# Half of a down-projection as three float32r products, with the low part finished by an adding transfer, and a last unit of work done by halves

## The reference, cut to what matters

```
attn = causal 7-tap filter over the sequence, softmaxed taps per head       # 8192 tokens x 192
h = attn @ moe_w_in                # 192 -> 2048
g = h * (1 / (1 + exp(-1.702 * h)))
x2 = g @ moe_w_out                 # 2048 -> 192
h = x2 @ moe2_w_in                 # 192 -> 2048
P = a0 + a1*h + a2*h^2 + a3*h^3
Q = 1 + |b0|*|h| + |b1|*h^2
out = (P / (Q + 1e-6)) @ moe2_w_out   # 2048 -> 192, float32
```

## Time and profile before

| | |
|---|---|
| device time, median of 3 | 1360.77 us (1360.70 to 1365.94) |
| the profiled execution's own time | 1360.97 us |
| its span in the trace | 1358.7 us |
| PE / DVE / ACT / POOL busy | 97 / 82 / 71 / 24 % |
| granted TensorE clock, mean | 0.995 |

### The profile page before, as it was taken

The page is one execution under the profiler, slowest core; times in us unless marked ns, Lnnn a source line. Parts: engine busy times, 40 slices in busy tenths (PEclk is TensorE's granted clock), DMA queues, the critical chain, the costliest instruction groups (busy, mean ns, idle before and its releaser), DMA issues. The chain is left out here.

```text
span 1358.7 us, 14959 instructions
## 1 busy us (share of the span) xinstructions
PE 1315.6 (97%) x4806; PEld 696.6 (51%) x4806; DVE 1115.3 (82%) x1225; ACT 967.3 (71%) x1145; POOL 323.0 (24%) x148
## 2 busy tenths in 40 slices
PE   5999999999999999999999999999999999999885
PEld 3445555555555555555555555555555555555441
DVE  4468888888888888888988888898888888877895
ACT  4357777777767777777777777777777777777684
POOL 2312222222222222222222222222222222222222
PEclk9999999999999999999999999999999999999899
DMA  7200000000000000000000000000000000000000
GB/s 191 73 0 12 1 12 13 1 24 1 12 13 0 23 0 24 0 12 12 0 24 0 23 0 12 13 0 23 0 24 1 12 1 0 13 1 12 0 12 12
DMA packets 32904, 20.55 MB, mean 15 GB/s; under 512 B 10321, under 2 KB 30801, under 8 KB 32849
## 3 DMA queue, kind: packets, MB, share of 16 engines
q1 hardware_dynamic: 32372, 19.93, 5.2%
q10 hardware_dynamic: 477, 0.01, 0.0%
HBM read 13.64 MB, written 6.29 MB: 15 GB/s over the span
## 5 line engine op out<-in xcount | busy, mean ns | idle before, releaser
L751 POOL TENSOR_TENSOR work<-work 128x1024 f32<-128x1024 f32 x128 | 303.3, 2370 | 987.4 <-ACT work L483 935.9
L284 PE MATMUL acc_a<-g,down 128*128 128x512 f32 x1024 | 476.6, 606 | 0.0
L284 PEld LDWEIGHTS acc_a<-g,down 128*128 128x128 f32 x1024 | 183.1, 189 | 291.7 <-issue 291.7
L290 PE MATMUL acc_b<-g,down 128*64 128x512 f32 x992 | 255.1, 606 | 17.6 <-DVE g L652 15.9
L641 DVE TENSOR_TENSOR work<-work,h 128x1024 f32<-128x1024 f32 x128 | 156.4, 1222 | 136.4 <-ACT work L483 135.6
L470 ACT ACTIVATE work<-h,par 128x1024 f32<-128x1024 f32 x128 | 142.7, 1115 | 173.9 <-PE h L278 172.8
L510 ACT ACTIVATE work<-work 128x1024 f32<-128x1024 f32 x128 | 135.9, 1062 | 157.2 <-POOL work L751 156.8
L270 PE MATMUL h<-x_a_hi,up_a_hi 128*128 128x512 f32 x512 | 234.5, 458 | 7.6 <-DVE x_a_lo L655 4.7
L271 PE MATMUL h<-x_a_lo,up_a_hi 128*128 128x512 f32 x512 | 201.3, 393 | 0.0
L272 PE MATMUL h<-x_a_hi,up_a_lo 128*128 128x512 f32 x512 | 200.9, 392 | 0.0
L273 PE MATMUL h<-x_b,up_b_hi 128*128 128x512 f32 x512 | 200.2, 391 | 0.0
(11 more groups left out here) (89 smaller groups left out, 961.0 us busy)
## 6 DMA issues: line engine op xcount, KB each, us to landing
out<-y_out SPq DMA_DIRECT2D x16, 384.0 KB, 2.5
x_in_a<-in_x SPq DMA_DIRECT2D x16, 256.0 KB, 2.8
down<-in_moe_w_out SPq DMA_DIRECT2D x8, 384.0 KB, 6.2
x_in_b<-in_x SPq DMA_DIRECT2D x32, 64.0 KB, 2.4
work<-in_moe_w_in SPq DMA_DIRECT2D x8, 256.0 KB, 4.4
work<-in_moe_w_in SPq DMA_DIRECT2D x16, 128.0 KB, 4.8
wts<-in_weight ACTq DMA_DIRECT2D x2, 0.4 KB
wts<-in_weight SPq DMA_DIRECT2D x2, 1.3 KB
```

Of the source, the lines that this page charges most:

```text
L284: last = mm(l.acc_a[:], l.down[:, f, 0:P], l.g[:, slot, k, :], start=f == 0, stop=f == STEPS - 1)
L290: return mm(acc_b[l.acc_row:l.acc_row + DB, :], l.down[:, f, P:D], l.g[:, slot, k, :], start=f == 0, stop=f == STEPS - 1)
L751: tt(m, sq[(s - LAG_RATIO) % 2], seed, ALU.mult).then_inc(m_ready, 1)
```

## The change

Three things change.

Layer 1's down-product into `acc_a` keeps its first unit (of the two in a duo) in float32, and makes of the second unit three float32r products. The weights' high part, its negative and the negative low part are made once. For the activations ACT makes, right after the function `g`, two copies of minus the rounded second unit, into `g_lo` and `g_nhi`. POOL then begins a transfer that adds the unrounded `g` onto `g_lo`, which leaves the low part there. A one-element multiply into `spare` stands ahead of the transfer on POOL. PE waits for that transfer before the first of these products. Tile 0's duos stay as they were.

The last duo of layer 2 is done in halves of 512 columns, with DVE in POOL's place for `m`, and `down_b` starts with the first half. Three idle matmuls stand on PE ahead of it.

The last tile's read-out is spread: `acc_b` is read as soon as it is done, DVE reads `acc_a`, the second half of the transposes has a bank of its own, DVE copies that half, and the store is two stores.

```diff
@@ pe
+            def down_a_split(d, slot):
+                acc = L1.acc_a[:]
+                mm(acc, L1.down[:, 2 * d, 0:P], L1.g[:, slot, 0, :], start=d == 0, stop=False)
+                mm(acc, down_nhi[:, d, :], g_nhi[:, slot, :], start=False, stop=False)
+                mm(acc, down_nlo[:, d, :], g_nhi[:, slot, :], start=False, stop=False)
+                return mm(acc, down_hi[:, d, :], g_lo[:, slot, :], start=False, stop=d == DUOS - 1)
...
-                    down_a(L1, e1, (s - LAG_DOWN1) % 2).then_inc(g1_used, 1)
+                    if isinstance(v1, int) and v1 < DUOS:
+                        down_a(L1, e1, (s - LAG_DOWN1) % 2).then_inc(g1_used, 1)
+                    else:
+                        slot = (s - LAG_DOWN1) % 2
+                        if isinstance(v1, int) and v1 == DUOS:
+                            pe.wait_ge(down_nlo_done, 1)
+                        pe.wait_ge(g_lo_done[slot], 16 * (4 * i + (s - LAG_DOWN1 - DUOS) // 2 + 1))
+                        down_a_split(e1, slot).then_inc(g1_used, 1)
...
+                if last(v2 + 1):
+                    for _ in range(3):
+                        mm(L1.acc_a[:], ident[:], xt_a[:, HALO:], start=True, stop=True)
@@ act
-                    fn(L1.g[:, (s - LAG_GELU) % 2, :, :], L1.h[:], ACT.Gelu_apprx_sigmoid).then_inc(g1_ready, 1)
+                    slot = (s - LAG_GELU) % 2
+                    fn(L1.g[:, slot, :, :], L1.h[:], ACT.Gelu_apprx_sigmoid).then_inc(g1_ready, 1)
+                    if not (isinstance(i, int) and i == 0):
+                        act.wait_ge(g1_ready, e + 1)
+                        fn(g_lo[:, slot, :], L1.g[:, slot, 1, :], ACT.Copy, scale=-1.0)
+                        fn(g_nhi[:, slot, :], L1.g[:, slot, 1, :], ACT.Copy, scale=-1.0).then_inc(g1_split, 1)
...
+                if last(v):
+                    act.wait_ge(z2_ready, v)
+                    for c in range(2):
+                        act.wait_ge(last_m, c + 1)
+                        fn(s1[:, c, :], m[:, c, :], ACT.Square, scale=root_c, bias=root_c * b1).then_inc(last_s1, 1)
...
+                    if i == 0 and s == DUOS - 2:
+                        fn(down_hi[:], L1.down[:, 1::2, 0:P], ACT.Copy).then_inc(down_hi_done, 1)
+                        fn(down_nhi[:], L1.down[:, 1::2, 0:P], ACT.Copy, scale=-1.0)
@@ dve
+                if last(v):
+                    dve.wait_ge(s2_ready, v)
+                    dve.wait_ge(seed_ready, v + 1)
+                    for c in range(2):
+                        tt(m[:, c, :], sk_last[:, c, :], seed[:, c, :], ALU.mult).then_inc(last_m, 1)
...
+                if isinstance(i, int) and i == 1:
+                    dve.wait_ge(down_hi_done, 1)
+                    tt(down_nlo[:], down_hi[:].bitcast(F32), L1.down[:, 1::2, 0:P], ALU.subtract)\
+                        .then_inc(down_nlo_done, 1)
@@ pool
+            def low_part(i, s):
+                n = i * DUOS + s
+                if live(n) and not (isinstance(i, int) and i == 0):
+                    pool.wait_ge(g1_split, n - DUOS + 1)
+                    wait(pool, spare_written, n - DUOS)
+                    tt(spare[:], ident[0:1, 0:1], ident[0:1, 0:1], ALU.mult).then_inc(spare_written, 1)
+                    pool.dma_start(g_lo[:, s % 2, :], L1.g[:, s % 2, 1, :], accum_op=ALU.add)\
+                        .then_inc(g_lo_done[s % 2], 16)
@@ sp
+                    if isinstance(i, int) and i == TILES + 1:
+                        sp.wait_ge(y_ready, 4 * (i - 1) - 2)
+                        sp.dma_start(dst[:, 0::2, :], y_out[:, 0::2, :]).then_inc(y_stored, 16)
+                        sp.wait_ge(y_last, 2)
+                        sp.dma_start(dst[:, 1::2, :], y_out[:, 1::2, :]).then_inc(y_stored, 16)
```

More of the change, by code:

```diff
@@ L146, in build_program @@
         ident = sb("ident", [P, P])
+        spare = sb("spare", [1, 1])
         wts = sb("wts", [P, 2, taps])
@@ L179, in alone, with last @@
             return isinstance(n, int) and n >= TOTAL
+        def last(duo):
+            return isinstance(duo, int) and duo == TOTAL - 1
         def h2_banks(n):
@@ L313, in transpose_y @@
                 wait(pe, acc2_read, 3 * (tile + 1))
+                ending = isinstance(tile, int) and tile == TILES - 1
+                bank = L2.h[:, 0, :] if ending and half else turned
                 for j in range(2):
-                    block = 2 * half + j
-                    nc.tensor.transpose(turned[:, j * P:(j + 1) * P], y_a[:, block * P:(block + 1) * P], ident[:])
-                nc.tensor.transpose(turned[:, 2 * P:3 * P], y_b[:, half * P:(half + 1) * P], ident[:])\
+                    block = half + 2 * j if ending else 2 * half + j
+                    nc.tensor.transpose(bank[:, j * P:(j + 1) * P], y_a[:, block * P:(block + 1) * P], ident[:])
+                nc.tensor.transpose(bank[:, 2 * P:3 * P], y_b[:, half * P:(half + 1) * P], ident[:])\
                     .then_inc(y_transposed, 1)
@@ L348, in step @@
                     wait(pe, x_evacuated, 2 * (i + 1 if not isinstance(i, int) else min(i + 1, TILES - 1)) + 2)
-                    wait(pe, y_ready, 4 * (i - 2) + 2 * half)
+                    if not (half and isinstance(i, int) and i == TILES + 1):
+                        wait(pe, y_ready, 4 * (i - 2) + 2 * half)
                     transpose_y(i - 2, half)
@@ L393, in step @@
                         wait(pe, acc2_read, 3 * (i - 1))
-                    pe.wait_ge(g2_ready, v2 + 1)
+                    if not last(v2):
+                        pe.wait_ge(g2_ready, v2 + 1)
                 for k in range(2):
                     if live(v2):
-                        down_b(L2, e2, (s - LAG_DOWN2) % 2, k)
+                        if last(v2):
+                            pe.wait_ge(last_g2, k + 1)
+                        last_b2 = down_b(L2, e2, (s - LAG_DOWN2) % 2, k)
+                        if last(v2) and k == 1:
+                            last_b2.then_inc(acc2_b_done, 1)
                     if live(v1):
@@ L498, in step @@
                     wait(act, y_stored, 16 * (i - 2))
[L499 to L502, removed]
+                    if isinstance(i, int) and i == TILES + 1:
+                        if half == 0:
+                            fn(y_out[:, 0::2, 0:P],
+                               turned[:, 0:2 * P].rearrange("p (j d) -> p j d", d=P), ACT.Copy).then_inc(y_ready, 1)
+                            fn(y_out[:, 0::2, P:D],
+                               turned[:, 2 * P:3 * P].rearrange("p (j d) -> p j d", d=DB), ACT.Copy)\
+                                .then_inc(y_ready, 1)
+                    else:
+                        fn(y_out[:, 2 * half:2 * half + 2, 0:P],
+                           turned[:, 0:2 * P].rearrange("p (j d) -> p j d", d=P), ACT.Copy).then_inc(y_ready, 1)
+                        fn(y_out[:, half::2, P:D],
+                           turned[:, 2 * P:3 * P].rearrange("p (j d) -> p j d", d=DB), ACT.Copy).then_inc(y_ready, 1)
                 if s == S_X1 and tile_live(i + 1):
@@ L519, in step @@
                 if s == S_ACC2 and tile_live(i - 2):
-                    act.wait_ge(g2_used, DUOS * (i - 1))
+                    ending = isinstance(i, int) and i == TILES + 1
+                    if ending:
+                        act.wait_ge(acc2_b_done, 1)
+                    else:
+                        act.wait_ge(g2_used, DUOS * (i - 1))
                     wait(act, y_transposed, 2 * (i - 2))
@@ L523, in step @@
                     fn(y_b[DB:P, :], acc_b[0:DB, HALF:NT], ACT.Copy).then_inc(acc2_read, 1)
-                    fn(y_a[:], L2.acc_a[:], ACT.Copy).then_inc(acc2_read, 1)
+                    if not ending:
+                        fn(y_a[:], L2.acc_a[:], ACT.Copy).then_inc(acc2_read, 1)
             act.wait_ge(halo_cleared, 1)
@@ L743, in step @@
                 v = n - LAG_RATIO
-                if live(v):
+                if live(v) and not last(v):
                     pool.wait_ge(seed_ready, v + 1)
```

50 lines of the change are left out of this document (44 added, 6 removed).

## The result

The changed kernel takes 1369.42 us (median of 6 runs, 1368.85 to 1380.11) against 1361.64 (6 runs): a ratio of 1.0062, 95% interval 1.0036 to 1.0087. It is slower by 0.6%, at the edge of what can be told. The run of 1380.11 us had a granted clock of 0.946, the five others 0.994 or more. Its profiled execution took 1368.85 us with a span of 1367.1, so the span grew by 8.4 us where the forecast put 3.7 on it.

What follows compares the result with a forecast made beforehand. PE, busy 97% of the span, was taken to bound the kernel. From 1361.0 us: 20.4 saved by products, 23.3 lost to stalls, 2.3 at step 0, 1 at the start, 2.5 saved at the end: 1365 us, range 1342 to 1396.

Steps and rivals of the forecast that it cites:

- The products: Layer 1's down-products on PE: one float32 product becomes three float32r, saving 0.17 us a duo, 20.4 us over 120 duos.
- ACT's copies: Two copies behind `g` delay ACT 1.22 us; PE stalls before transposes in three steps a tile, 23.3 us lost.
- DVE is the bound there: Step 0: `down_b` waits for DVE's `g`, so a PE 0.17 us quicker waits; 15 x 0.15 = 2.3 us lost.
- It is hidden: POOL's transfer onto `g_lo`: taken as 4 to 5 us, with 6.1 in hand before PE needs it; no cost.
- Start and end: First split duos lose 1 us (0 to 4); the end by halves and spread read-out saves 2.5 us (1 to 4).
- The sum: Whole kernel: 1361.0 - 20.4 + 23.3 + 2.3 + 1 - 2.5 = 1364.7, so 1365 us.
- The copies come in time: Rival on ACT: stalls before transposes go and the gain is left, 1341 us, or 1352 with half the stalls; chance 0.22.
- The late transfer: Rival: PE stops at the head of layer 1's `down_a` in every step, about 1400 us; chance 0.21.
- the held POOL: Rival: `spare` stands back for a DVE instruction, so POOL begins the transfer 1.2 us later; priced 1395 us; chance 0.08.
- the cost of changing back: Rival on PE: float32 after float32r takes 0.15 us, leaving 0.02 gain a duo, 1383 us; chance 0.07.

Runs made afterwards that it cites:

- e3: Changed kernel without split products and transfer; ACT still makes both copies, which nothing reads: 1372.78 us, ratio 1.0072.
- e1: Changed kernel with ACT's two copies moved behind the copies out of `turned`, still ahead of `split_x1` and the squares: 1359.14 us, ratio 0.9969.
- e4: Changed kernel with the three float32r products but no copies in the loop and no transfer, second unit using wrong data: 1343.17 us, ratio 0.9852.
- e7: e6 with the read-out of `acc_b` and `acc_a` moved ahead of the reciprocal's seed on ACT: 1342.75 us, ratio 0.9854.
- e2: Kernel before with only the changed kernel's new end; no split product, copies or transfer: 1357.4 us, ratio 0.9959.
- e8: Changed kernel without the transfer and `spare`; products read `g_lo` as ACT wrote it: 1363.82 us, ratio 1.0006.
- e9: e7 without the transfer and `spare`; products read `g_lo` as ACT wrote it: 1338.98 us, ratio 0.9824.
- e6: e1 with the copies at their old place in tile 1 and `split_x1`'s three small copies behind the squares in step 6: 1346.14 us, ratio 0.9886.
- e10: e7 with DVE's loop over pairs of tiles written out, the other engines keeping their loops: 1334.67 us, ratio 0.979.
- e5: Changed kernel with the `spare` multiply ahead of the transfer made 128x1024 elements instead of one: 1436.75 us (one round), ratio 1.0548.

## Why the prediction was nearly right, and where it was wrong

The forecast was 1365 us, with slower as the likeliest outcome (0.47), and the result 1369.4. Its main mechanism was shown; two terms were missing.

*The products* bring 0.17 a step where PE sets the time (9.83 to 9.66, steps 2 and 3), and the change of format costs nothing either way. Right.

*ACT's copies.* 1.22 us later, as worked out. Stalls of 0.46, 0.62 and 0.62 where 0.58, 0.58 and 0.63 stood; e3 brings them back alone and e1 takes them away. Right, also in that a late DVE `g` of step 7 hides behind them (e1: 0.79).

*"DVE is the bound there"*, one step with 0.15 lost. In an ordinary tile it is that: 1 to 2 stays at 9.90 against 9.89, since the 0.15 between DVE's end and PE's start in the earlier trace rows is the signal's way and no margin. But the same kind of bound stood in step 4 too, where `down_b` waits for ACT's read-out of layer 2. I did not look for it, since no wait of the first rank pointed there. A small one did, in the waits of the kernel before:

```profile
PEld acc_b L290 <- ACT y_a L524: 5.7, 11, 1.8
```

It costs 0.08 + 0.17 = 0.25 a tile, 3.5 us in all; e4 shows it without copies and e7 takes it away.

*"It is hidden"*, of the transfer, is the step that failed. For PE it was right: it lands in 3.2 us, less than the 4 to 5 taken, and no matmul in the loop waits for it. (By the Trainium skill, DMA: Bandwidth & Descriptors, Anatomy of one DMA — SWDGE (gpsimd) path, a plain one would take 2.6, an estimate. The adding one took 3.2; no plain one ran.) But I weighed only who waits for its data, and not who shares the DMA engines with it. With it the loads of x and DVE's start at the head of the loop are late: 1369.42 against 1363.82 without it, and 1342.75 against 1338.98.

*Start and end.* The first `m` starts at 90.46 us (90.66 before), so the start costs nothing. At the end of the changed kernel, in DVE, PE and SP:

```profile
1352.95 1.28 DVE L728 TENSOR_TENSOR work<-work 128x512 f32<-128x512 f32 x2
...
1355.58 2.74 PE L457 MATMUL acc_a<-xt_a,ident 128*128 128x512 f32 x6
...
1358.25 1.93 PE L319 MATMUL acc_b<-g,down 128*64 128x512 f32 x4
...
1362.96 0.41 PE L347 MATMUL turned<-ident,y_a 128*128 128x128 f32 x2 [0.87 <-DVE y_a L759]
...
1364.10 0.37 SPq L267 DMA_DIRECT2D out<-y_out  x1
```

From the last `m` to `down_b` 5.30 us (6.07 in the earlier trace rows; forecast a gain of 1.2, got 0.8), held by the idle matmuls as said. To the first store 11.15 against 13.83: 2.7 saved, forecast 2.5. The medians of e2 say more (5.5), which no row explains.

*The sum.* Forecast for a tile: -1.36 + 1.79 + 0.15 = +0.58; measured +1.00. The difference of 0.42 is 0.25 in step 4, 0.18 in 0 to 1, 0.08 in 1 to 2 and -0.09 in the stalls. The 0.26 of steps 0 and 1 are the heads: without the transfer (e8) these two steps are 0.19 and 0.30 shorter. Against the kernel before it looks like less, since its heads lost 0.62 in 1 to 2 already. In e8 this loss is hidden by the stall before step 0; in e9, which has no such stall, 0.47 of it is back.

*The rivals.* "The copies come in time" (1341 to 1352) did not happen, but it is what e6, e7 and e10 make of it by ACT's order. The late transfer, the held POOL (`spare` starts at 608.43, at once behind `m`) and the cost of changing back did not happen either. What a transfer that lands e us late costs was not tried: e5 was too blunt for it, because it stopped DVE.

## What to carry to other kernels

When work is added to an engine that has slack, look at what stands behind it in every step, not in the common one: the slack was behind the copy that another engine waited for, and three steps of eight paid. When the bounding engine is made faster, list for every step what it waits for with no time in hand; steps with no margin return none of the gain, whatever the mean says. A transfer whose data come in time can still cost, since it slows the others on the same DMA engines, and among these are the instructions of an engine that jumps back in a loop.

## What the runs showed of the hardware that I had not expected

- Behind a jump back DVE can wait for its own instructions. What shows it: entries of the queue of kind "instruction" behind each of the four jumps, DVE's start 2.4 to 2.9 us behind the last of them in five kernels, and both gone when DVE's loop is written out. That the entries hold DVE's code is inferred from this. It need not show as issue: in the kernel before, the profile put such a wait down to PE, which had been done for 0.74 us. Writing DVE's loop out took that queue from 40 packets (e7) to 26, and 7 us off the loop.
- A multiply of POOL on 128x1024 elements (1.88 us) and DVE's L722, with two inputs from SBUF, don't overlap: 2.83 us instead of 1.22. L719 and L721, which read `h` straight from where PE wrote it, run beside POOL's `m` in their usual 1.22 and 1.28 (606.05 and 607.31 in the changed kernel, `m` from 606.10 to 608.47).
- A transfer of 256 KB from SBUF to SBUF that adds, begun by POOL, held POOL for 0.80 us and landed in 3.2. With it in the kernel, loads of 256 and 64 KB on SP's queue took 4.4 and 4.1 us, without it (e8) 2.8 and 2.5. In e7, where the same transfers fall otherwise, they took 3.2 and 3.9.
